# A mixture-of-experts kernel on one core: a weight load placed behind a gather, and the order of the tail steps of routing

## The reference, cut to what matters

```python
e = fresh_e if (s == 0 or local_gate[b, s] < 0.5) else prev_e
h = np.maximum(x[b, s] @ w1[e], 0.0)
out[b, s] = p[e] * (h @ w2[e])
```

## Time and profile before

| | us |
|---|---|
| median of 3 runs | 288.93 |
| lowest, highest | 288.07, 289.92 |
| profiled execution, its own time | 290.14 |
| its span, first to last instruction | 288.4 |
| TensorE busy | 265.5 (92%) |
| VectorE busy | 194.0 (67%) |
| ScalarE busy | 131.5 (46%) |
| GpSimd busy | 59.9 (21%) |

### The profile page before, as it was taken

The page is one execution under the profiler, slowest core; times in us unless marked ns, Lnnn a source line. Parts: engine busy times, 40 slices in busy tenths (PEclk is TensorE's granted clock), DMA queues, the critical chain, the costliest instruction groups (busy, mean ns, idle before and its releaser), DMA issues.

```text
span 288.4 us, 4986 instructions
## 1 busy us (share of the span) xinstructions
PE 265.5 (92%) x1913; PEld 226.2 (78%) x1913; DVE 194.0 (67%) x393; ACT 131.5 (46%) x238; POOL 59.9 (21%) x57
## 2 busy tenths in 40 slices
PE   8599999998798299999999999999999999999980
PEld 3488888886695199898888888888889889889860
DVE  1345998987566025769878959859958968867600
ACT  1023536364542113555565833754845745753310
POOL 0553343430003110210320330250150050011011
PEclk9999999999899755899999999999999999999997
DMA  7999999812003510370891880990792782520010
GB/s 236 390 415 410 410 415 420 334 63 90 36 0 115 250 60 0 84 306 1 343 365 39 323 363 4 324 371 6 291 343 82 286 305 109 216 111 28 1 36 29
DMA packets 11512, 57.75 MB, mean 200 GB/s; under 512 B 1758, under 2 KB 1886, under 8 KB 9696
## 3 DMA queue, kind: packets, MB, share of 16 engines
q1 hardware_dynamic: 7200, 46.94, 42.2%
q0 software_dynamic: 2560, 7.34, 6.7%
q10 hardware_dynamic: 1728, 3.15, 2.9%
HBM read 51.13 MB, written 7.34 MB: 203 GB/s over the span
## 4 chain that ended last, share of the span: by engine, by line
PE 79%; DVE 7%; DMA 6%; issue 2%; ACT 2%; SPq 1%; POOL 0%; POOLq 0%
PE ps L983 22%; PE ps L985 10%; PE ps L1003 10%; PE ps L1002 10%; PE ps L1004 10%; DMA qkv_sb<-qkv 3%; DMA x_gathered<-x_rows,gather_idx 3%; PE ps L916 3%; PE ps L883 3%; PE ps L963 3%; PE ps L871 3%; PE ps L906 2%; PE ps L947 2%; PE ps L894 2%; DVE scores_masked L673 1%
## 5 line engine op out<-in xcount | busy, mean ns | idle before, releaser
L983 PE MATMUL ps<-x_sorted_T,w_split 128*128 128x480 f32 (+1 forms) x288 | 96.5, 394 | 2.0 <-issue 1.4
L985 PE MATMUL ps<-x_sorted_T,w_split 128*128 128x240 f32 (+1 forms) x288 | 78.6, 273 | 0.0
L693 DVE TENSOR_TENSOR w_split<-w_raw,w_split 128x1024 fp32r<-128x1024 f32 x56 | 66.2, 1220 | 9.8 <-ACT w_split L460 9.8
L983 PEld LDWEIGHTS ps<-x_sorted_T,w_split 128*128 128x128 f32 x288 | 59.2, 205 | 9.4 <-issue 2.5
L706 DVE TENSOR_REDUCE h_sums<-ps 128x240 f32<-128x480 f32 (+1 forms) x72 | 43.0, 599 | 32.6 <-PE ps L985 31.9
L985 PEld LDWEIGHTS ps<-x_sorted_T,w_split 128*128 128x128 f32 x288 | 59.7, 207 | 0.3
L460 ACT CAST w_split<-w_raw 128x1024 fp32r<-128x1024 f32 x56 | 55.8, 1040 | 8.0 <-DMA w_raw<-w 8.0
L469 ACT ACTIVATE hT<-h_sums 128x240 fp32r<-128x240 f32 (+1 forms) x72 | 27.4, 381 | 65.0 <-DVE h_sums L706 65.0
L1002 PE MATMUL ps<-w_split,hT 128*128 128x512 f32 x128 | 52.1, 407 | 0.0
L1003 PE MATMUL ps<-w_split,hT 128*128 128x512 f32 x128 | 51.0, 398 | 0.0
L1004 PE MATMUL ps<-w_split,hT 128*128 128x512 f32 x128 | 50.9, 397 | 0.0
(11 more groups left out here) (108 smaller groups left out, 251.1 us busy)
## 6 DMA issues: line engine op xcount, KB each, us to landing
w_raw<-w SPq DMA_DIRECT2D x14, 2048.0 KB, 9.2
qkv_sb<-qkv SPq DMA_DIRECT2D x22, 512.0 KB, 13.0
w_raw<-w SPq DMA_DIRECT2D x8, 512.0 KB, 15.4
x_rows<-x_rows_sb ACTq DMA_DIRECT2D x12, 256.0 KB, 6.3
c_attn_sb<-c_attn SPq DMA_DIRECT2D x1, 548.0 KB, 5.7
qkv_sb<-qkv SPq DMA_DIRECT2D x2, 256.0 KB, 14.3
ident_and_w_router<-ident_router SPq DMA_DIRECT2D x1, 274.0 KB, 8.1
c_attn_sb<-c_attn SPq DMA_DIRECT2D x1, 256.0 KB, 7.3
```

Source lines behind the costliest of these rows:

```text
L693: V.tensor_tensor(ws[:, par, 1, half, at:at + PIECE], raw[:, half, at:at + PIECE], ws[:, par, 0, half, at:at + PIECE].bitcast(fp32), ALU.s ...
L983: MM(at[:, 0:2 * w].rearrange("p (a t) -> p a t", a=2), ws[:, par, 0, 0, cols], xTs[:, k, :, sub], start=(k == 0), stop=(k == KD - 1), ski ...
L985: last = MM(at[:, w:2 * w], ws[:, par, 1, 0, cols], xTs[:, k, 0, sub], start=False, stop=(k == KD - 1), skip_group_check=True)
```

## The change

It has four parts.

1. SP waits, before it loads w2 of expert 1, also until the gather of expert 0's second half has landed (`xg_in[1]`).
2. VectorE computes the rest of `gather_idx` after `h_add(0, 5)`, before `h_lo(0, 5)`, instead of behind `h_lo(0, 7)`.
3. `route_e` is cut in two; its second comparison is now `route_f`. For group 2 in the tail `x_lo(0, 0)` stands between the two.
4. The order of the tail: on TensorE `up(0, 2)` stands ahead of `table(2)`, `down(0, 0)` ahead of `table(3)`, `down(0, 4)` ahead of the product for the ends, and the broadcast product stands behind `x_transpose(0, 1)`. On VectorE `e0_low(7)` stands behind the count steps instead of ahead of them.

```diff
                         sp.wait_ge(e0_split, (half + 1) * PIECES)
+                        if half == 1:
+
+                            sp.wait_ge(xg_in[1], 16)
...
             route_e(GROUPS - 2)
             x_lo(0, 0)
+            route_f(GROUPS - 2)
             route_a(GROUPS - 1)
...
             route_e(GROUPS - 1)
+            route_f(GROUPS - 1)
             h_lo(0, 4, 0, 1)
-            for f in range(5, KF):
+            h_add(0, 5, 1)
+
+            dve.wait_ge(tab_added, GROUPS)
+            V.tensor_scalar(gather_idx[:, 1:], tab_ps[:, 0, 1:], -1.0, 0.0, ALU.add, ALU.max).then_inc(table0, 1)
+            h_lo(0, 5, 0, 1)
+            for f in range(6, KF):
                 h_add(0, f, 1)
                 h_lo(0, f, 0, 1)
-            dve.wait_ge(tab_added, GROUPS)
-            V.tensor_scalar(gather_idx[:, 1:], tab_ps[:, 0, 1:], -1.0, 0.0, ALU.add, ALU.max).then_inc(table0, 1)
-            e0_low(2 * PIECES - 1)
...
             k.did(V.tensor_reduce(nov[:, :], ovm[:, :], AX.X, ALU.add))
+            e0_low(2 * PIECES - 1)
...
             to_rows(GROUPS - 1)
+            up(0, 2, 0, 0, 1)
             table(GROUPS - 2)
-            up(0, 2, 0, 0, 1)
...
+            down(0, 0, 0, 0)
             table(GROUPS - 1)
-            down(0, 0, 0, 0)
             down(0, 1, 0, 0)
...
             down(0, 3, 0, 0)
+            down(0, 4, 0, 0)
             pe.wait_ge(dm, DM_STEPS["overflows"])
             MM(small_ps[0:NE, 1:2], through, nov[:, :], start=True, stop=True).then_inc(pm, 1)
-            down(0, 4, 0, 0)
-            down(0, 5, 0, 0)
+            for f in range(5, KF):
+                down(0, f, 0, 0)
+            x_transpose(0, 1)
             pe.wait_ge(dm, DM_STEPS["past"])
             MM(small_ps[:, 8:8 + 2 * NOV], ones[0:NE, :], past[:, :, :].rearrange("p a u -> p (a u)"),
                start=True, stop=True).then_inc(pm, 1)
-            down(0, 6, 0, 0)
-            down(0, 7, 0, 0)
-            x_transpose(0, 1)
```

More of the change, by code:

```diff
@@ L656, in route_e, with route_f @@
                                       col_f[:, :].unsqueeze(2).to_broadcast([P, GC, CT]), ALU.is_equal))
+            def route_f(g):
+                k = Steps(dve, dr, g * RD, DR["match"])
+                dve.wait_ge(tab_added, g)
                 k.did(V.tensor_tensor(row_oh[:, :, :], iota_row.unsqueeze(1).to_broadcast([P, GC, P]),
@@ L727, in _ @@
                     route_e(g - 2)
+                    route_f(g - 2)
                 if m == NC + GC:
```

## The result

| | before | changed |
|---|---|---|
| median, us | 289.43 (4 runs) | 278.76 (4 runs) |
| lowest, highest | 288.07, 290.63 | 276.67, 280.84 |
| the same two programs in a later set of runs (e5) | 289.2 (11 runs) | 276.6 (6 runs, 275.02 to 280.64) |
| profiled execution: time, span | 290.14, 288.4 | 280.84, 279.0 |
| TensorE busy | 265.5 | 262.2 |

The ratio is 0.9609 with a 95% interval of 0.9501 to 0.9716; in the later set of runs (experiment e5) it is 0.9524, 0.9471 to 0.9578. The change is faster by 4 to 5%. These and all later ratios compare the means of the runs within 1.5% of the same kernel's fastest, so a kernel's slowest group is in part left out of them, while its median is over all its runs. The forecast was 275.0, and its range (272.8 to 283.5) holds both medians.

What follows compares the result with a forecast made beforehand. TensorE was taken to bound the kernel, so an earlier expert 1 moves the end. The terms, 8.2 + 0 + 7.1 = 15.3 us off 290.14, gave 274.8; forecast 275.0, range 272.8 to 283.5.

Steps and rivals of the forecast that it cites:

- What bounds the kernel, and what happens if the second half ends earlier: TensorE bounds the seven back-to-back experts; ending expert 0's second half earlier moves the end by as much.
- (a): Expert 0's first half, around table(2): up(0, 4) starts at 78.6 instead of 81.46, 2.9 us gained.
- (b): Gather index to second half's transposes: these start at 90.15 instead of 98.30, 5.3 us beyond (a), 8.2 in all.
- (c): Second half's transposes to up(1, 0): 2.45 us against 2.50 before, nothing gained or lost, TensorE idle about 1.8 us.
- (d): From the second half's eight up to expert 1: clock kept at 2.4 GHz, 7.1 us gained, charges for split and gather included.
- the first rival: Clock falls at the pause ahead of up(1, 0), most of the eight up at 1.2 GHz: 281 to 282 us; chance 0.27.
- (e): SP's new wait ahead of loading w2 of expert 1: only later weight loads queue behind it, no cost.
- slow by itself: Rival: the second half's gather takes 8.93 us even without w2 beside it, giving 286.0 us; chance 0.06.
- the end moved: Denies the rival that a gather or w1's split holds expert 1 where it was: 288.9 us; chance 0.04.
- no run was slower: Denies the rival that the clock stays low through the 24 down and expert 1's up: 296.3 us; chance 0.03.

Runs made afterwards that it cites:

- e5: Changed kernel once more with no edit, in a later set of runs; 276.6 us, ratio 0.9524.
- e7: Changed kernel with the first reorder undone: table(2) ahead of up(0, 2), second comparison ahead of x_lo; 285.32 us, ratio 0.9736.
- e10: Kernel before with the first reorder alone: up(0, 2) ahead of table(2), x_lo ahead of the second comparison; 288.74 us, ratio 0.9895.
- e1: Kernel before with only SP's wait for the second half's gather ahead of loading w2 of expert 1; 278.25 us, ratio 0.9534.
- e11: Kernel before with only the gather index moved behind h_add(0, 5); 279.15 us, ratio 0.9523.
- e2: Changed kernel without SP's wait for the gather ahead of loading w2; 275.96 us, ratio 0.9492.
- e6: Changed kernel with the second half's transposes and broadcast product between down(0, 5) and down(0, 6); 274.21 us, ratio 0.9474.
- e12: Kernel before with 22 unneeded matmuls in TensorE's 4.04 us wait for the gather; 283.44 us, ratio 0.9748.
- e4: Kernel before with 16 unneeded matmuls in TensorE's 4.04 us wait for the gather; 291.76 us, ratio 0.9969.
- e8: Changed kernel with the gather index back behind h_lo(0, 7); 283.31 us, ratio 0.9776.
- e3: Changed kernel with six unneeded matmuls in the pause ahead of up(1, 0); 276.7 us, ratio 0.9525.
- e9: Kernel of e6 with the slot values of group 2 earlier on ScalarE; 273.37 us, ratio 0.9358.

## Why the prediction was right, and where it was off

**What bounds the kernel, and what happens if the second half ends earlier.** Right: the gain at the start of expert 1 (14.9) arrived whole at the end.

**(a) The start.** The sum had `up(0, 4)` at 78.6; it came at 78.79 and 78.98 in the two profiles. The wait ahead of `table(2)` was 0.77 us (0.6). As a price the 2.9 us was nearly right for these two executions (2.7 and 2.5) and too small in general. Undoing the part cost 7.6 in the one pair of executions that compare (e7), since the clock can also stay low for 13 us there; doing it alone in the kernel before took away its slowest group of runs (e10).

**(b) The gather.** Right in place and size: index 84.66 (84.5), gather issued at 85.55 to 85.7 (85.3), landed after 3.5 (3.6), the split of the last piece the new wait of 0.38 (0.4), transposes from 90.4 and 90.6 (90.15), so that (a) and (b) together gave 7.9 and 7.7 us of the 8.2. But the prediction let parts 1 and 2 stand beside each other without asking whether one would do. e1, e11 and e2 answer: either is enough, and in the changed kernel the wait on SP is idle.

**(c) Transposes to `up(1, 0)`.** Right: 2.4 us, with 1.74 of idleness (1.8). That the broadcast behind the transposes puts VectorE's chain ahead of `x_lo` showed as L806 to L820 from 91.31 to 92.1 and `x_lo` at 92.25. I priced it at nothing gained or lost and did not ask whether it had to be there; e6 shows that moving two `down` behind the transposes is worth some 2.4 us in the median, of which 1.1 is the pause; the rest is that four of e6's six runs are of its fastest group, and only two of e5's six.

**(d) The clock.** This is the step that was off, as a single value. Eight `up` at 7.16 (7.3) and the split of w1 late by 0.58 (0.3) were right for the runs with no fall, and the gather amid w2 cost nothing: issued 2.6 us behind the load, it landed after 5.8 us, not 8.93. The term was 7.1, and e12 has 6.9 for the clock alone. But only two of ten runs took that course. Five had a short fall (276.6 to 277.0), which neither the forecast nor a rival held, because the prediction looked for falls only from 72 us on (see below); three had the first rival's (280.5 to 280.8 against 281 to 282). In the profiled one of these the clock fell at 94.7, behind 1.74 us of idleness with dense work on both sides, so dense work did not always keep it up. I gave the first 0.60 and the second 0.27 as if one of them were true of the kernel, where each was a share of its runs. The median then is a number between: 1.6 over the forecast in one set of runs, 3.8 in the other.

**(e) The new wait.** Right that it costs nothing; wrong to let it stand as part of what brings the gain in this order (e2).

**The other rivals** fell: the gather was not slow by itself (3.4 to 3.7 us in e1, e2, e5, e11 against 8.9 to 10.4 wherever w2 was issued beside it), the end moved, and no run was slower.

How far the median lay from the forecast is in part luck: four of these ten runs can have their median anywhere from 276.0 to 280.6, all of it inside the range.

What stays open: where the short fall of the middle group lies is not shown, since no profiled execution of the changed kernel is of that group. But four of the fourteen profiled executions (e4, e6, e8, e11) have one of some 3.5 us, between 14.5 and 19.1 us, behind a wait of 1.9 to 2.0 us for q, k and v (e1 and e10 have such a wait and no fall). It cost 1.56 us in e6 and e11, which is the distance of the middle group from the first (276.7 against 275.2 in the mean), and by an estimate from its length it takes 0.006 off the mean clock, about the step from 0.993 or 0.994 to 0.987. If that is the fall, it lies in a part that the change does not touch. Open, too, is why three of ten runs fall at a pause of the same 1.74 us while the others don't. That the pause has a part in it is supported by counting, not shown in one trace: of the 14 runs with it (the changed kernel and e2) four are above 280; of the 18 with it filled or covered (e3, e6, e9) none is above 278.

## What to carry to other kernels

When a small transfer on the critical path lands late, look what large one is issued within a microsecond of it before touching its own engine; then either issue the small one earlier or hold the large one back, and test whether one of the two is enough. Count a hole on TensorE not by its length but by what stands behind it: here one of 1.6 us was followed in two of six traces by 13 us of back to back work at 1.2 GHz, which each time cost over 5 us. Where a program's runs fall in groups with different mean clocks, forecast the groups and their shares, look through the whole program for the falls and not only where the change is, and take the spread as a thing to be removed: the best version was found by closing holes of 0.8 to 1.7 us. And compare executions of the same course before a difference of medians is put down to an edit.

## What the runs showed of the hardware that was not expected

- TensorE's clock stayed at 1.2 GHz through 10 to 11 us of back to back `up` matmuls (94.7 to 105.0 in the profiled execution of the changed kernel, 78.0 to 89.0 in e7) and 13.7 in the kernel before, and was back 1.1 to 2.1 us after the first `down`. The same program takes the fall in one run and not in the next.
- With the short wait of 1.0 us in e8 and the pause of 1.7 behind it the mean clock was low in four runs of four; with the pause alone four of 14 were above 280 us.
- The gather beside w2 took 8.9 and 9.1 us in the kernel before and e10, but 10.4 in e4 and e12, where TensorE worked beside it instead of waiting. Nothing in the traces says why. Issued 2.6 us behind w2 instead of 0.9 ahead of it, the next gather took 5.8 us in e5 and 6.6 in the changed kernel's first profile.
- VectorE's split beside POOL's issue of the gather lengthened that issue: 1.00 us without it, 1.21 with 0.3 us of overlap (e1), 1.77 with 0.9 (before, e4, e8, e10, e12).
